# Attention with top-1 experts on one core: scores ordered by thirds of the keys, the row maximum taken in two parts

## What is computed

```python
q_pool = q.reshape(B, H, S // 2, 2, D).mean(axis=3)
scores = (1.0 / np.sqrt(D)) * np.matmul(q_pool, k.transpose(0, 1, 3, 2))
scores = scores - np.max(scores, axis=-1, keepdims=True)
attn = np.exp(scores)
attn = attn / (np.sum(attn, axis=-1, keepdims=True) + 1e-09)
out = np.matmul(attn, v)          # then a routed mixture of experts on out
```

## Time and profile before

| | us |
|---|---|
| median of 3 runs | 947.26 (945.54 to 947.38) |
| the profiled execution, its own time | 944.8 |
| its span, first to last instruction | 943.0 |
| PE busy in the span | 885.9 (94%) |
| DVE busy | 433.1 (46%) |
| ACT busy | 325.2 (34%) |
| POOL busy | 315.0 (33%) |
| the 144 row maxima (L622) | 195.4, 1358 ns each |
| PE busy between 60 and 540 us, the steady part of attention | 465.0 of 480 |

### The profile page before, as it was taken

The page is one execution under the profiler, slowest core; times in us unless marked ns, Lnnn a source line. Parts: engine busy times, 40 slices in busy tenths (PEclk is TensorE's granted clock), DMA queues, the critical chain, the costliest instruction groups (busy, mean ns, idle before and its releaser), DMA issues. The chain is left out here.

```text
span 943.0 us, 13344 instructions
## 1 busy us (share of the span) xinstructions
PE 885.9 (94%) x4970; PEld 594.6 (63%) x4971; DVE 433.1 (46%) x597; ACT 325.2 (34%) x530; POOL 315.0 (33%) x334
## 2 busy tenths in 40 slices
PE   5899999999999999999999956999999999999997
PEld 5677777778777877877787735444444444444443
DVE  4786666657566665656575554121111112111111
ACT  2555655645565555546555510010000101000010
POOL 7563365346436634643560001011111111111110
PEclk7999999999999999999999975999999999999999
DMA  9524443352434234343501058733064700101110
GB/s 221 131 63 108 108 115 81 89 134 68 108 106 125 66 97 125 83 109 91 131 9 39 14 191 292 270 139 113 34 216 154 251 33 33 33 24 34 34 33 17
DMA packets 49278, 97.17 MB, mean 103 GB/s; under 512 B 24015, under 2 KB 24015, under 8 KB 49232
## 3 DMA queue, kind: packets, MB, share of 16 engines
q1 hardware_dynamic: 45472, 85.51, 32.0%
q0 software_dynamic: 3760, 11.02, 3.5%
HBM read 87.07 MB, written 10.75 MB: 104 GB/s over the span
## 5 line engine op out<-in xcount | busy, mean ns | idle before, releaser
L622 DVE TENSOR_REDUCE negmax<-psum 128x1 f32<-128x1152 f32 x144 | 195.4, 1358 | 109.0 <-PE psum L383 92.3
L383 PE MATMUL psum<-kstack,qstack 128*128 128x384 f32 x768 | 171.1, 359 | 8.7 <-DVE kstack L295 5.2
L408 PE MATMUL psum<-ident,probs 128*128 128x128 f32 x1152 | 160.7, 275 | 18.9 <-DVE x_out L656 13.9
L522 ACT ACTIVATE probs<-psum,negmax 128x1152 f32<-128x1152 f32 x128 | 156.5, 1222 | 49.5 <-DVE negmax L622 45.6
L936 PE MATMUL psum<-wbuf,xgT 128*128 x368 | 163.5, 597 | 1.9 <-DVE xgT L1094 1.1
L953 PE MATMUL psum<-wbuf,hT 128*128 x368 | 161.8, 592 | 1.1 <-DVE hT L1102 1.1
L408 PEld LDWEIGHTS psum<-ident,probs 128*128 128x128 f32 x1152 | 134.1, 142 | 32.4 <-DVE x_out L656 21.3
L383 PEld LDWEIGHTS psum<-kstack,qstack 128*128 128x128 f32 x768 | 131.3, 193 | 23.8 <-ACT probs L522 12.0
L517 ACT ACTIVATE pT<-psum 128x512 f32<-128x512 f32 x160 | 95.3, 595 | 117.8 <-PE psum L408 117.8
L936 PEld LDWEIGHTS psum<-wbuf,xgT 128*128 128x128 f32 x368 | 68.7, 192 | 80.4 <-issue 80.4
L953 PEld LDWEIGHTS psum<-wbuf,hT 128*128 128x128 f32 x368 | 68.1, 190 | 78.3 <-issue 78.3
(11 more groups left out here) (164 smaller groups left out, 773.2 us busy)
## 6 DMA issues: line engine op xcount, KB each, us to landing
wbuf<-in_w SPq DMA_DIRECT2D x64, 512.0 KB, 4.4
qraw<-in_q_t SPq DMA_DIRECT2D x64, 288.0 KB, 5.0
kraw<-in_k_t SPq DMA_DIRECT2D x64, 288.0 KB, 5.6
vraw<-in_v_t SPq DMA_DIRECT2D x16, 576.0 KB, 4.7
x_rows<-x_out SPq DMA_DIRECT2D x32, 128.0 KB, 2.0
x_rows<-x_out SPq DMA_DIRECT2D x32, 16.0 KB, 1.8
xg<-x_rows,src_now POOLq DMA_INDIRECT x24, 3.6
out<-y,dst_now POOLq DMA_INDIRECT x23, 2.8
```

The lines of the kernel that those rows point to most:

```text
L383: last = nc.tensor.matmul(dst[:, third, 0:THIRD], qstack[p % 2][:, part, tile_cols(side, i)], kstack[p % 2][:, side, third * THIRD:(third ...
L408: last = nc.tensor.transpose(dst[:, i * P:(i + 1) * P], probs[side][:, i, c * P:(c + 1) * P], ident[:])
L522: nc.scalar.activation(probs[side][:, i, :].rearrange("p (a b) -> p a b", a=3), slot(f, i)[:, :, 0:THIRD], ACT.Exp, bias=negmax[:, p % 2, ...
L622: nc.vector.tensor_reduce(negmax[:, p % 2, col:col + 1], slot(f, i)[:, :, 0:THIRD], AX.XY, ALU.max, negate=True).then_inc(max_ready, 1)
```

## The change

The loops of `score` and `score_tail` change places: the thirds are now outside and the parts inside, so both (in the tail, all four) matmuls of a third come one after the other. After the second third a new semaphore, `two_thirds`, is raised.

`take_max` has three instructions instead of one. DVE waits for `two_thirds`, and reduces the first two banks (768 columns) into one column of a new small tile, `part_max`. It waits for `ring_full` and reduces the last bank (384 columns) into the other column. It waits for its own `max_parts`, and an elementwise minimum of the two negated maxima (`tensor_tensor`, 128 x 1, both inputs and the output in on-chip memory) gives `negmax`. The numbers are the same.

```diff
+    part_max = sb("part_max", [P, 2, 2])
...
+    two_thirds, max_parts = sem("two_thirds"), sem("max_parts")
...
-            for part in range(2):
-                for third in range(3):
+            for third in range(3):
+                for part in range(2):
                     last = nc.tensor.matmul(dst[:, third, 0:THIRD], qstack[p % 2][:, part, tile_cols(side, i)],
                                             kstack[p % 2][:, side, third * THIRD:(third + 1) * THIRD],
                                             start=(part == 0), stop=(part == 1))
+                if third == 1:
+                    last.then_inc(two_thirds, 1)
             last.then_inc(ring_full, 1)
...
-            for n, (side, part) in enumerate([(0, 0), (0, 1), (1, 0), (1, 1)]):
-                for third in range(3):
+            for third in range(3):
+                for n, (side, part) in enumerate([(0, 0), (0, 1), (1, 0), (1, 1)]):
...
+                if third == 1:
+                    last.then_inc(two_thirds, 1)
             last.then_inc(ring_full, 1)
...
             col = TAILTILE if i == "tail" else side * FULL + i
+            n = QT * p + col + 1
+            dve.wait_ge(two_thirds, n)
+            nc.vector.tensor_reduce(part_max[:, n % 2, 0:1], slot(f, i)[:, 0:2, 0:THIRD], AX.XY, ALU.max, negate=True)
             wait_round(dve, f, i)
-            nc.vector.tensor_reduce(negmax[:, p % 2, col:col + 1], slot(f, i)[:, :, 0:THIRD], AX.XY, ALU.max, negate=True).then_inc(max_ready, 1)
+            nc.vector.tensor_reduce(part_max[:, n % 2, 1:2], slot(f, i)[:, 2, 0:THIRD], AX.X, ALU.max, negate=True).then_inc(max_parts, 1)
+            dve.wait_ge(max_parts, n)
+            tt(negmax[:, p % 2, col:col + 1], part_max[:, n % 2, 0:1], part_max[:, n % 2, 1:2], ALU.min).then_inc(max_ready, 1)
```

## The result

The changed kernel took 974.48 us in the median of 4 runs (969.64 to 976.34), against 946.4 for the kernel before (4 runs set beside it): a ratio of 1.0289, with a 95% interval from 1.0248 to 1.033. The forecast was 984, the range 950 to 1000. The profiled execution took 976.34 us, its span is 974.5, 31.5 more than that of before.

A forecast was written before the change was run, and what follows sets the result against it. The DVE chain up to x_out was taken to set each attention phase. Minima waiting for POOL, 34.0 us, plus 2.6 us where POOL is idle, made 36.6 us on 947.26: 984 us, range 950 to 1000.

The forecast's parts named there:

- The bound: Attention: DVE's chain from maximum 0 to x_out, 5.39 us, sets the phase; PEld waited 21.3 us for x_out.
- PE's order at nothing: Score matmuls on PE: two in a row adding into one bank cost nothing; six still take 1.00 us.
- The split: take_max on DVE: three instructions take 1.64 us against 1.36; x_out 0.16 us later in 16 phases, 2.6 us.
- The minimum waits for POOL: Odd phases on DVE: the two-input minimum waits out POOL's running instruction, as L295 did; 34.0 us over 15 phases.
- The prices of the two orders: x_out in odd phases: 3.06 us later if POOL starts before the first minimum, 1.00 us if DVE does.
- the signs that the prediction named for being right: Odd phases: minima over 1 us for tiles 0 and 1, x_out 8 us and more after maximum 0; even phases within 0.2.
- How often POOL comes first: First minimum against L288 in odd phases: POOL first in 8 of 13, DVE in 5, averaging 2.27 us a phase.
- The clock: Rival: after POOL-first pauses PE's grant falls to 1.2 GHz, up to 45 us more, 1029 us; chance 0.07.
- The start and the end: Odd phases 1 and 3 were taken like the other 13, with less ground, at 2.27 us each.
- The chances: Whole kernel: forecast 0.75, one column slipping past 0.14, faster 0.04, clock 0.07; measured slower 0.89, within 0.08, faster 0.03.
- rival 1: Minimum beside POOL: one column slips past as L588 did, leaving 0.16 us in 31 phases, 5 us, 952; chance 0.14.

The follow-up runs named there:

- the experiment with the pointer: Changed kernel with the minimum as a tensor_scalar, one part as tensor input, the other as per-partition scalar, both in on-chip memory: 957.14 us, ratio 1.0104.
- the kernel without a head start: Changed kernel with the first part of the maximum waiting for ring_full instead of two_thirds: 1018.45 us, ratio 1.0738.

## Why the prediction was right, and where it was off

**The bound.** Right. The chain on DVE up to `x_out` sets the phase, shown from both sides: it grew and the time grew, and with `x_out` out of it the time fell by 1.3%. One reading was too narrow: the wait for `x_out` is not PE's only one in every phase. PEld's loads of a score also waited for exponentials, 29 times and 6.8 us in all between 50 and 545 us, and that wait stayed when `x_out` had been moved away.

**PE's order at nothing.** Right, measured by itself at 0.9991.

**The split, 0.28 us a tile, and 0.16 us a phase where POOL is idle.** Right within hundredths: 952 and 546 ns against 956 and 555, and 5.88 against 5.72 us. The kernel with the first part in PSUM, in which nothing else is left of the change, is 5.0 us slower than the kernel before, and 31 x 0.16 is 5; but its trace has 0.14 a phase and 1.9 us at the start. A single tile costs a little less than predicted, since its minimum is done 1.62 us after the first part starts: 0.26 more than the one reduction, not 0.28.

**The minimum waits for POOL.** Right, and shown by moving one column to PSUM. The choice between L295 and L588 as the nearest kin was the right one for the `tensor_tensor`; the experiment with the pointer shows that L588 too told the truth, for one column of a `tensor_scalar`.

**The prices of the two orders.** 3.06 us predicted, 3.12 found (8.84 - 5.72) with POOL first; 1.00 predicted, 0.95 found with DVE first. But the signs that the prediction named for being right (over 1 us for tiles 0 and 1, `x_out` 8 us and more after maximum 0) came only in the 3 POOL-first phases; in the other 10 `x_out` came 6.3 us after the old place of maximum 0.

**How often POOL comes first.** This is the term that was mis-sized. I put the request of the first minimum 1.15 us after the old maximum 0 and counted 8 of 13 phases. It comes 1.46 us after the first part, which is 1.11 after the old maximum's start: the second part was 0.01 shorter and the handover 0.03 instead of 0.05, and the first part started 0.02 earlier. The distances of L288 run from 1.06 to 1.17: in 8 of the 13 phases of the kernel before it is 1.13 or less, but in only 4 it is 1.11 or less, so 0.04 us halves the count. In the profiled execution those with L290 1.47 us or more after the first part are DVE first (10), those with 1.45 or less POOL first (3). With 3 and 10 the sum's 29.5 us for these phases would have been 19.2, and the whole 36.6 some 26.

**The clock.** I held its fall to be a rival with 0.07, priced at up to 3 us a phase. Between 60 and 540 us it fell, after the POOL-first phases alone, at 1.3 to 1.6 us each: 4.6 us of the profiled execution. The prediction had named a grant below 1.00 there as its sign of being wrong, and no row stood behind its price of some 3 us. What I leaned on, a pause of 3.4 us with a grant of 1.00, was a poor guide: the grant had only just risen, and a like pause at the same place in the kernel with the part in PSUM was followed by a fall. One pause at full clock says nothing certain of the next. One POOL-first phase of the kernel without a head start passes without a fall.

**The start and the end.** The 3.2 us ahead of the `x_out` of phase 2 and the 1.7 of phase 3 stand beside 4.5 in the sum (2 x 2.27), which did not work them out. The kernel with the part in PSUM has 1.9 us ahead of phase 2 too, without a single wait for POOL; the clock differs there, as shown, and no experiment parts the two. The 1.3 us behind the last `x_out` say nothing of the change: the experts, which no version changes, took from 390.5 to 395.7 us in the profiled executions.

**The chances.** They don't quite add up: the forecast and the clock have 0.82 together, and most of rival 1's 0.14 on top is over the 0.89 given for slower.

Two errors thus partly cancelled: too many phases with POOL first, 10.3 us too much, and no price for the clock, 4.6 us too little. 36.6 - 10.3 + 4.6 is 30.9, beside the 31.5 of the span. That the time lies inside the forecast's own 965 to 996 is not luck, since the right count alone would have given 947.3 + 26.3 = 973.6. That the number missed by only 9.5 us owes something to the clock. And how often POOL came first in the other three runs behind the median is not known.

## What to carry to other kernels

Splitting a reduction to overlap its first part with the producer pays only where the consumer is idle when the first part is ready, and then the gain is the head start less the cost of the extra instructions: here 0.35 less 0.26 us, about 0.1 a phase in the trace of the kernel that splits only there, and too little to show in its time. Before adding a small instruction with two inputs in on-chip memory on DVE, look at what POOL is doing at that time: the small one can last as long as POOL's large one, and moving an input to PSUM takes that away. Where two engines ask for the same thing within hundredths of a microsecond in every period, predict both outcomes and their prices, not an average.

## What the runs showed of the hardware that was not expected

- One column is enough to wait: a `tensor_tensor` of 128x1 with both inputs in on-chip memory took up to 2.47 us beside POOL instead of 0.16. With one input in PSUM it took 0.158, and as a `tensor_scalar` with the second value as per-partition scalar 0.21, both beside a busy POOL; but a `tensor_scalar` of five columns from on-chip memory took 0.83 in the mean in that same run, beside POOL.
- The race is sharp. The minimum asked for at 1.46 us won against a POOL start at 1.47 and lost against one at 1.45.
- The granted clock fell to 1.2 GHz after PE had been 77% busy for 3.3 us and 31% for 2.1 us more (2.54 of 3.30 and 0.66 of 2.10 in the rows above), while in the kernel before it had stayed at 2.4 GHz through 3.4 us of almost nothing. In the kernel with the part in PSUM it did fall after a like pause at the same place.
